# Three edits in the last stage of a fused attention and two-layer MLP kernel: a group of output stores ahead of weight loads, two VectorE steps exchanged, eight semaphores made four

## The chip, the cores and the metric

One core of a Trainium2 chip. The metric is the device time of one launch in microseconds (us), the median of some runs. In the profile PE is TensorE (PEld its weight loads), DVE is VectorE, ACT is ScalarE, POOL is GpSimd and SP is SyncE, which here only issues DMAs.

## The reference

All arrays are float32. Attention with a soft cap feeds a leaky MLP, which feeds a gated MLP with an RMS norm:

```python
# q, k, v: (2, 12, 448, 64)
scores = cap * np.tanh((q @ k.T) / np.sqrt(64) / cap)
attn = softmax(scores) ; x = (attn @ v) as (896, 768)
h = x @ w_in                                   # 768 -> 2048
x = np.maximum(0.01 * h, h) @ moe_w_out        # 2048 -> 768
xn = x / sqrt(mean(x * x, -1) + 1e-6) * rms_g
g, val = xn @ w_gate, xn @ w_val               # 768 -> 1536 each
out = (g * sigmoid(g) * val) @ w_out2          # 1536 -> 768
```

## The kernel before

Activations are kept transposed (features on the 128 partitions, the 448 tokens of one batch element in a row). Each product of a pair of weight row blocks with the two batch elements is done by a seven-product scheme of the Strassen kind: products named P1, P5, P7, P6, P3, P2 and P4, each on a half of the contraction. Every float32 product is made of three matmuls on a high and a low part of each operand (`w_hi` with `z_high`, `w_hi` with `z_low`, `w_lo` with `z_high`). One product of the last stage is so 3 x 3 = 9 matmuls of 128x128 weights on 448 columns.

The way of a weight: SP loads a raw block of 384 KB into one of four slots `w_raw` (`load_raw`); a slot is free when GpSimd has made the low part of the last weight that uses the old block (`raw_free`, a wait on `w_lo_done`). Products P1, P2 and P4 use the raw block as it is. The others use a sum or difference that DVE makes in `s_sum` (`s_part`, lines 1018 to 1027). ACT copies the weight to `w_hi` (line 686), GpSimd subtracts it from the original into `w_lo` (line 576), and PE waits for `w_lo_done` before the product. There are seven slots for finished weights.

The last stage, out = act @ w_out2, has three units, called `UNITS`, `UNITS + 1` and `UNITS + 2` in the code, and first, second and third unit here. Each makes two row blocks of the output for both batch elements. The second and the third have 14 products (seven for each half of the 1536 features); they use the banks of PSUM by turns, the third those of the first. DVE drains a unit by `take_p5`, `take_p7` and `take_p6` and by four results, `result_11`, `result_12`, `result_21` and `result_22`, in the buffers `sq0`, `sq1`, `u2` and `a_t`, from which SP stores them (`store`, line 551, 224 KB each).

Every engine runs its instructions in the order in which the code writes them, and the DMAs of loads and stores are all issued from SP, whose waits are in that same order: a DMA behind a wait is not issued before the wait is over. Nothing moves them at build time. `load_last(s)` issues a unit's four raw blocks (`w_raw` slots 0, 1, 2, 3), and before the change the end of SP's order is `load_last` of the three units and then `store` of the three. `z_lower(1, T4)` is three subtractions for the low part of the operand of the second unit's very last product (P4 of the second half). PE's order of a 14-product unit is P1, P5, P7, P6, the same four for the second half, and then P3, P2 and P4 (P3, P4 and P2 in the third unit), each for both halves.

Of the kernel before, what the change touches and what calls it, by code (L numbers as in the profile page):

```python
# [11 lines left out]
def at_least(eng, sem, value):  # L12

    if value > 0:
        eng.wait_ge(sem, value)


def build(nc, qk, v, cap, w_in, w_out, w_gate, w_val, w_out2, rms_g, out, recips):
    PAIRS, _, QK = qk.shape
# [8 lines left out]
    KH = KD // 2  # L28
# [13 lines left out]
    B11, T1, T3, T2, B22, B21, T4, B12 = range(8)  # L42
# [3 lines left out]
    UNITS = U1 + N2  # L46
# [29 lines left out]
    def raw_of(s):  # L76
        if s >= UNITS:
            return RAW_LAST + 4 * (s - UNITS)
        return 2 * s if s < U1 else 2 * U1 + STEPS // 2 + 2 * (s - U1)
# [10 lines left out]
    with ExitStack() as ctx:  # L90
# [71 lines left out]
        def sem(name):  # L162
            return ctx.enter_context(nc.semaphore(name))
# [10 lines left out]
        recip_out = sem("recip_out")  # L174
        recip_row_in = [sem(f"recip_row_in{s}") for s in range(2)]
        raw_in = [sem(f"raw_in{s}") for s in range(4)]
        out_sem = [[sem(f"out_stored{s}_{u}") for u in range(2)] for s in range(4)]

        ident_done = sem("ident_done")
        consts = sem("consts")  # L180
# [70 lines left out]
        def cols(i, n=S):  # L251
            return slice(i * n, i * n + n)

        def tiles(t, n):
            return t.rearrange("p (t c) -> p t c", c=n)
# [163 lines left out]
        O11, O12, O21, O22 = range(4)  # L419
# [41 lines left out]
        @block.sync  # L461
        def _(sp):
            def load_qk(p):

                at_least(sp, qk_hi_done, p - 1)
                at_least(sp, qk_lo_done, p - 1)
                c = slice(FIRST if p == 0 else 0, QK)
                sp.dma_start(qk_raw[p % 2][:, c], qk[p][:, c]).then_inc(qk_in[p % 2], 16)

            def load_v(p):  # L470

                at_least(sp, pv_done, p - 1)
                if p < 2:
                    sp.wait_ge(v_ones_set, p + 1)
                sp.dma_start(tiles(v_ones[p % 2][:, :], 128)[:, :, 0:D], v[p]).then_inc(v_in[p % 2], 16)

            def spread_sums(p):

                sp.wait_ge(x_raw_done, p + 1)
                at_least(sp, eps_done, p - 1)  # L480
                sp.dma_start(sums[p % 2][:, :],
                             x_raw[p % 2][D:D + 1, :].rearrange("o (p j) -> o p j", p=128)).then_inc(sums_in, 16)

            def store_recip(p):
                sp.wait_ge(recip_done, p + 1)
                sp.dma_start(recips[p].rearrange("(p j) -> p j", p=128), recip[p % 2][:, :]).then_inc(recip_out, 16)

            def load_recip_row(p):

                sp.wait_ge(recip_out, 16 * (p + 1))  # L490
                at_least(sp, x_norm_done, 2 * (p - 1))
                sp.dma_start(recip_row[p % 2][HEAD[0], :],
                             recips[p].partition_broadcast(D)).then_inc(recip_row_in[p % 2], 16)

            def raw_free(r):

                if RAW_OUT <= r < raw_of(U1):
                    sp.wait_ge(w_lo_done, W_OUT + 2 * (r - RAW_OUT) + 2)
                elif r < RAW_LAST:
                    s = r // 2 if r < RAW_OUT else U1 + (r - raw_of(U1)) // 2  # L500
                    sp.wait_ge(w_lo_done, widx(s, P4) + 1)
                else:
                    s, k = divmod(r - RAW_LAST, 4)
                    last = [(P2, 0), (P4, 0), (PB, 1), (PD, 1)][k] if s == 0 else ((P2, P4)[k % 2], k // 2)
                    sp.wait_ge(w_lo_done, widx(UNITS + s, *last) + 1)

            def load_raw(r, src):
                if r >= 4:
                    raw_free(r - 4)
                n = src.shape[-1]  # L510
                sp.dma_start(w_raw[r % 4][:, 0:n], src).then_inc(raw_in[r % 4], 16)

            sp.dma_start(qk_raw[0][:, 0:FIRST], qk[0][:, 0:FIRST]).then_inc(first_in, 16)
            load_qk(0)
            sp.wait_ge(first_in, 16)
            load_v(0)
            load_qk(1)
            load_qk(2)
            load_v(1)
            load_qk(3)  # L520
            for p in range(PAIRS):
                spread_sums(p)
                if p + 2 < PAIRS:
                    load_v(p + 2)
                if p + 4 < PAIRS:
                    load_qk(p + 4)
                if p < 4:
                    load_raw(p, w_in[p])
                store_recip(p)
                load_recip_row(p)  # L530
            sp.dma_start(rms_col[:, :], rms_g.rearrange("(c p) -> p c", p=128),
                         allow_slow_non_contiguous=True).then_inc(gains_in, 16)
            for r in range(4, RAW_OUT):
                load_raw(r, w_in[r])
            for k in range(STEPS // 2):
                load_raw(RAW_OUT + k, w_out[k])
            for f in range(N2):
                load_raw(raw_of(U1 + f), w_gate[f])
                load_raw(raw_of(U1 + f) + 1, w_val[f])

            def load_last(s):
                m, r = s - UNITS, raw_of(s)
                for k, (row, part) in enumerate(((m, 0), (m + KH, 0), (m, 1), (m + KH, 1))):
                    load_raw(r + k, w_out2[row, part])

            def store(s):
                for kind in RESULTS[s - UNITS]:
                    row, b, tile, scaled = result(s, kind)
                    row = s - UNITS + KH * row
                    sp.wait_ge(scaled, s - UNITS + 1)  # L550
                    sp.dma_start(out[row * 128:(row + 1) * 128, cols(b)], tile[:, :]).then_inc(out_sem[kind][(s - UNITS) % 2], 16)

            load_last(UNITS)
            load_last(UNITS + 1)
            load_last(UNITS + 2)
            store(UNITS)
            store(UNITS + 1)
            store(UNITS + 2)
            for kind in range(4):
                sp.wait_ge(out_sem[kind][0], 32)  # L560
                sp.wait_ge(out_sem[kind][1], 16)

        @block.gpsimd
        def _(pool):
# [375 lines left out]
        def _(dve):  # L940
# [95 lines left out]
            def take_p5(s):  # L1036

                dve.wait_ge(p1_kept, s + 1)
                dve.wait_ge(prod_done, count[widx(s, P5, last_part(s))])
                if s == LAST - 1:  # L1040
                    dve.wait_ge(out_sem[O22][0], 16)
                dve.tensor_tensor(a_t[s % 2][:, :], bank(s, BANK_C), p1[s % 2][:, :], ALU.add).then_inc(a_done, 1)

            def take_p7(s):

                dve.wait_ge(a_done, s + 1)
                dve.wait_ge(prod_done, count[widx(s, P7, last_part(s))])
                dve.tensor_tensor(a_t[s % 2][:, :], bank(s, BANK_D), a_t[s % 2][:, :], ALU.add).then_inc(a2_done, 1)

            def take_p6(s):  # L1050
                dve.wait_ge(prod_done, count[widx(s, P6, last_part(s))])
                if s == LAST - 1:
                    dve.wait_ge(out_sem[O21][0], 16)
                dve.tensor_tensor(u2[s % 2][:, :], bank(s, BANK_B), p1[s % 2][:, :], ALU.add).then_inc(u2_done, 1)


# [267 lines left out]
            def z_lower(part, blk):  # L1324
                for c in range(KH):
                    z_lo(part, blk, c)
# [12 lines left out]

            def result_11(s):  # L1340
                dve.wait_ge(act_done, 2 * N2)
                if s > UNITS:
                    dve.wait_ge(out_sem[O11][(s - 1 - UNITS) % 2], 16)
                wait_result(s, P2, PB)
                dve.tensor_tensor(sq[0][:, :], bank(s, BANK_A), r_bc[:, cols(0)], ALU.mult).then_inc(o11_done, 1)

            def result_12(s):
                dve.wait_ge(act_done, 2 * N2)
                dve.wait_ge(u2_done, s + 1)
                if s > UNITS:  # L1350
                    dve.wait_ge(out_sem[O12][(s - 1 - UNITS) % 2], 16)
                wait_result(s, P3, PB)
                dve.tensor_tensor(sq[1][:, :], bank(s, BANK_C), u2[s % 2][:, :], ALU.add).then_inc(c12_done, 1)
                dve.wait_ge(c12_done, s + 1)
                dve.tensor_tensor(sq[1][:, :], sq[1][:, :], r_bc[:, cols(1)], ALU.mult).then_inc(o12_done, 1)
# [15 lines left out]
            s = U1  # L1371
# [40 lines left out]
            s = UNITS - 1  # L1412
# [19 lines left out]
            s = UNITS  # L1432
# [22 lines left out]
            s_part(s + 1, P3, 1)  # L1455
            take_p5(s + 1)
            take_p7(s + 1)
            take_p6(s + 1)
            z_lower(1, T4)
            result_11(s)  # L1460
            result_12(s)
            result_21(s)
# [1 line left out]
            s = UNITS + 1  # L1464
# [8 lines left out]
            s = UNITS + 2  # L1473
# [362 lines left out]
```

## Time and profile before

| | us |
|---|---|
| three runs | 566.59, 568.21, 570.43 |
| median | 568.21 |
| profiled execution, its own time | 568.21 |
| its span in the profile | 566.4 |
| PE busy in the span | 561.6 |

The span is what the engines and queues show. The profiled execution took 568.21 us, 1.8 us more than its span, and it is also the median. So a time predicted from the trace is the span's change added to 568.21. The rows below use times from the start of the span. A group of an answer that merges several instructions (x3) shows one duration from the first one's start to the last one's end.

### The profile page before, as it was taken

How to read it: one execution, taken by the hardware profiler on the slowest of the kernel's cores; microseconds unless marked ns; L12 is line 12 of the kernel's file. 1: busy time of each engine (PE TensorE's matmuls, PEld its weight loads, DVE VectorE, ACT ScalarE, POOL GpSimd, SP SyncE). 2: the span in 40 equal slices, each digit the busy share in tenths (PEclk: the TensorE clock that was granted, in tenths of full speed). 3: DMA queues.
4: the chain of work that ended last, by engine and by line, in shares of the span. 5: the costliest groups of instructions: out<-in, count | busy, mean ns of one | idle time of the engine just before them, and what ended most of it. 6: DMA issues, size and time to landing. Idle time of an engine off the chain costs nothing.

```text
span 566.4 us, 7857 instructions
## 1 busy us (share of the span) xinstructions
PE 561.6 (99%) x2706; PEld 472.0 (83%) x2706; DVE 413.7 (73%) x575; ACT 294.4 (52%) x513; POOL 313.8 (55%) x272
## 2 busy tenths in 40 slices
PE   9999999999999999999999999999999999999997
PEld 5544554688999999999999999999999999998896
DVE  4468897685545455324985499999999999999963
ACT  6889888226444464434644456444334445825330
POOL 1026464479656652234853469767766897526672
PEclk9999999999999999999999999999999999999999
DMA  6355332123111142110211011111221111120511
GB/s 171 97 174 162 110 113 52 49 57 112 57 56 57 56 130 66 57 45 23 75 54 57 1 57 57 56 57 56 77 89 59 56 57 58 56 57 0 171 73 65
DMA packets 29720, 41.49 MB, mean 73 GB/s; under 512 B 17009, under 2 KB 18673, under 8 KB 29681
## 3 DMA queue, kind: packets, MB, share of 16 engines
q1 hardware_dynamic: 29536, 40.99, 23.0%
q8 instruction: 22, 0.36, 0.3%
q14 instruction: 18, 0.14, 0.1%
q10 hardware_dynamic: 144, 0.00, 0.0%
HBM read 38.15 MB, written 2.80 MB: 72 GB/s over the span
## 4 chain that ended last, share of the span: by engine, by line
PE 91%; DVE 4%; issue 3%; DMA 1%; ACT 0%; POOL 0%; DVEq 0%; ACTq 0%
PE ps L1579 46%; PE ps L1646 21%; PE ps L1514 9%; PE ps L1743 8%; PE ps L1502 4%; PE ps L1520 2%; PE ps L1506 1%; DVE act_lo L1321 1%; DVE x_lo L1321 1%; PE ps L1588 1%; DMA sums<-x_raw 1%; DVE x_raw L955 0%; DVE s_sum L1024 0%; POOL w_lo L576 0%; PE ps L1698 0%
## 5 line engine op out<-in xcount | busy, mean ns | idle before, releaser
L576 POOL TENSOR_TENSOR w_lo<-w_raw,w_hi 128x384 fp32r<-128x384 f32 x111 | 131.1, 1189 | 140.3 <-ACT w_hi L686 139.6
L1579 PE MATMUL ps<-x_hi,w_hi 128*128 128x448 f32 x420 | 154.9, 369 | 0.0
L1579 PE MATMUL ps<-x_hi,w_lo 128*128 128x448 f32 x420 | 154.1, 367 | 0.0
L1579 PE MATMUL ps<-x_lo,w_hi 128*128 128x448 f32 x420 | 154.0, 367 | 0.0
L576 POOL TENSOR_TENSOR w_lo<-s_sum,w_hi 128x384 fp32r<-128x384 f32 x100 | 113.6, 1149 | 69.5 <-ACT w_hi L686 69.5
L686 ACT ACTIVATE w_hi<-s_sum 128x384 fp32r<-128x384 f32 x100 | 51.2, 523 | 91.6 <-PE ps L1579 53.3
L1579 PEld LDWEIGHTS ps<-x_hi,w_hi 128*128 128x128 f32 x420 | 79.0, 188 | 8.4 <-issue 1.3
L1579 PEld LDWEIGHTS ps<-x_hi,w_lo 128*128 128x128 f32 x420 | 78.9, 188 | 7.0
L1579 PEld LDWEIGHTS ps<-x_lo,w_hi 128*128 128x128 f32 x420 | 79.0, 188 | 6.7
L686 ACT ACTIVATE w_hi<-w_raw 128x384 fp32r<-128x384 f32 x111 | 56.3, 514 | 11.8 <-PE ps L1579 7.2
L1514 PE MATMUL ps<-probs,v_ones 128*65 128x448 f32 x144 | 56.6, 541 | 0.2 <-DVE x_raw L955 0.2
L662 ACT ACTIVATE probs<-ps,capc 128x896 f32<-128x896 f32 (+1 forms) x48 | 42.0, 901 | 12.2 <-PE ps L1502 10.8
L1514 PEld LDWEIGHTS ps<-probs,v_ones 128*65 128x65 f32 x144 | 19.3, 137 | 30.3 <-issue 29.1
L669 ACT ACTIVATE probs<-probs,capc 128x1344 f32<-128x1344 f32 (+2 forms) x25 | 41.1, 1644 | 0.8
L1132 DVE TENSOR_TENSOR x_lo<-g,x_hi 128x448 fp32r<-128x448 f32 x32 | 22.1, 736 | 23.5 <-ACT x_hi L718 23.5
L1132 DVE TENSOR_TENSOR ring_lo<-g,ring_hi 128x448 fp32r<-128x448 f32 x32 | 24.6, 812 | 15.2 <-ACT ring_hi L718 15.2
L1027 DVE TENSOR_TENSOR s_sum<-w_raw,s_sum 128x384 f32<-128x384 f32 x25 | 26.2, 1049 | 5.7 <-POOL w_lo L576 3.5
L1743 PE MATMUL ps<-act_lo,w_hi 128*128 128x448 f32 x84 | 29.9, 368 | 0.0
L1018 DVE TENSOR_TENSOR s_sum<-w_raw 128x384 f32<-128x384 f32 x25 | 23.2, 929 | 7.4 <-DMA w_raw<-in_w_in 6.4
L718 ACT ACTIVATE ring_hi<-g 128x448 fp32r<-128x448 f32 x32 | 16.6, 569 | 22.5 <-PE ps L1646 22.5
L718 ACT ACTIVATE x_hi<-g 128x448 fp32r<-128x448 f32 x32 | 16.6, 570 | 21.8 <-PE ps L1646 21.8
L1646 PE MATMUL ps<-ring_hi,w_lo 128*128 128x448 f32 x96 | 27.5, 368 | 0.0
(182 smaller groups left out, 1047.2 us busy)
## 6 DMA issues: line engine op xcount, KB each, us to landing
w_raw<-in_w_out SPq DMA_DIRECT2D x28, 384.0 KB, 3.1
w_raw<-in_w_in SPq DMA_DIRECT2D x16, 384.0 KB, 3.8
qk_raw<-in_qk SPq DMA_DIRECT2D x11, 480.0 KB, 4.3
w_raw<-in_w_gate SPq DMA_DIRECT2D x12, 384.0 KB, 3.0
w_raw<-in_w_val SPq DMA_DIRECT2D x12, 384.0 KB, 3.6
v_ones<-in_v SPq DMA_DIRECT2D x12, 224.0 KB, 3.3
recip_row<-recips SPq DMA_DIRECT2D x12, 224.0 KB, 3.3
out<-sq SPq DMA_DIRECT2D x6, 224.0 KB, 1.9
```

The costliest lines, as they stand in the source:

```text
L576: pool.tensor_tensor(w_lo[:, c], source, w_hi[:, c].bitcast(F32), ALU.subtract).then_inc(w_lo_done, 1)
L662: act.activation(tiles(probs_of(p, i, n), S), ps[:, bank_of(p, i):bank_of(p, i) + n, 0:S], ACT.Tanh, scale=capc[:, 4:5]).then_inc(tanh_don ...
L669: act.activation(c, c, ACT.Exp, scale=capc[:, 2:3], bias=capc[:, 6:7]).then_inc(exp_done, 1)
L686: act.activation(w_hi[:, c], w_source(n), ACT.Copy).then_inc(w_hi_done, 1)
L718: act.activation(ring(i, b, ring_hi, x_hi), g_tile(2 * f + b), ACT.Copy).then_inc(g_hi_done, 1)
L1018: dve.tensor_tensor(dst, m2[:, lower], m2[:, upper], ALU.add).then_inc(s_done, 1)
L1027: dve.tensor_tensor(dst, m1[:, upper], s_sum[:, cols(2, HALF)], ALU.subtract).then_inc(s_done, 1)
L1132: dve.tensor_tensor(ring(i, b, ring_lo, x_lo), g_tile(2 * f + b), ring(i, b, ring_hi, x_hi).bitcast(F32), ALU.subtract).then_inc(g_lo_done, 1)
L1514: pe.matmul(ps[0:D + 1, pv_bank(p) + h, 0:S], v_ones[p % 2][:, c:c + D + 1], probs[p % 2][:, (2 * t + h) * S:(2 * t + h + 1) * S], start=( ...
L1579: last = pe.matmul(ps[:, base(s) + BANK_OF[j], 0:S], w[:, w_c], x[:, xs(j, c)], start=(j in (P1, P5, P7, P6) and c == 0 and w is w_hi and ...
L1646: last = pe.matmul(ps[:, ROW_BANK[m] + b, 0:S], w[:, w_c], ring(i, b, beside, in_x), start=(f == 0 and w is w_hi and x == "hi"), stop=(f = ...
L1743: last = pe.matmul(ps[:, base(s) + BANK_OF[j], 0:S], w[:, w_c], x(part, j, c), start=(j in (P1, P5, P7, P6) and part == 0 and c == 0 and w ...
```

## The change

1. In SP's order, `store(UNITS)`, the four output stores of the first unit, now stands between `load_last(UNITS + 1)` and `load_last(UNITS + 2)`, ahead of the third unit's four raw loads.
2. In DVE's order, `z_lower(1, T4)` now stands before `take_p6(s + 1)`.
3. The semaphores of the stores, two for each of four kinds of result, are one for each kind, which counts up; the waits are for 16, 32 or 48 on it, and the last one of SP is four waits, where it was eight.

```diff
-        out_sem = [[sem(f"out_stored{s}_{u}") for u in range(2)] for s in range(4)]
+        out_sem = [sem(f"out_stored{s}") for s in range(4)]
...
-                    sp.dma_start(out[row * 128:(row + 1) * 128, cols(b)], tile[:, :]).then_inc(out_sem[kind][(s - UNITS) % 2], 16)
+                    sp.dma_start(out[row * 128:(row + 1) * 128, cols(b)], tile[:, :]).then_inc(out_sem[kind], 16)
...
             load_last(UNITS)
             load_last(UNITS + 1)
+            store(UNITS)
             load_last(UNITS + 2)
-            store(UNITS)
             store(UNITS + 1)
             store(UNITS + 2)
             for kind in range(4):
-                sp.wait_ge(out_sem[kind][0], 32)
-                sp.wait_ge(out_sem[kind][1], 16)
+                sp.wait_ge(out_sem[kind], 16 * KH)
...
                 if s == LAST - 1:
-                    dve.wait_ge(out_sem[O22][0], 16)
+                    dve.wait_ge(out_sem[O22], 16 * (s - 1 - UNITS))
...
                 if s == LAST - 1:
-                    dve.wait_ge(out_sem[O21][0], 16)
+                    dve.wait_ge(out_sem[O21], 16 * (s - 1 - UNITS))
...
             def result_11(s):
                 dve.wait_ge(act_done, 2 * N2)
-                if s > UNITS:
-                    dve.wait_ge(out_sem[O11][(s - 1 - UNITS) % 2], 16)
+                at_least(dve, out_sem[O11], 16 * (s - UNITS))
...
             take_p7(s + 1)
+            z_lower(1, T4)
             take_p6(s + 1)
-            z_lower(1, T4)
             result_11(s)
```

SP's queue near its end, the change against the kernel before. `w_raw_51` to `w_raw_54` are the raw slots 0 to 3 (the first two rows end the second unit's loads, the unmarked four are the third unit's), `sq_67`, `sq_68`, `u_0_62` and `a_t_60` hold the first unit's results 11, 12, 21 and 22:

```order
 L511 DMA w_raw_53<-in_w_out 128x768
 L511 DMA w_raw_54<-in_w_out 128x768
+L551 DMA out<-sq_67 128x448
+L551 DMA out<-sq_68 128x448
+L551 DMA out<-u_0_62 128x448
+L551 DMA out<-a_t_60 128x448
 L511 DMA w_raw_51<-in_w_out 128x768
 L511 DMA w_raw_52<-in_w_out 128x768
 L511 DMA w_raw_53<-in_w_out 128x768
 L511 DMA w_raw_54<-in_w_out 128x768
-L551 DMA out<-sq_67 128x448
-L551 DMA out<-sq_68 128x448
-L551 DMA out<-u_0_62 128x448
-L551 DMA out<-a_t_60 128x448
```

The four stores moved ahead of the four loads; each store has a wait for its own result.

DVE's order in the second unit, before, from `take_p5` of the second unit (line 1042) over the results of the first to the first weight sum of the third unit (line 1018):

```order
L1042 TENSOR_TENSOR a_t_61<-ps,p_1_59 128x448 [waits prod_done,p1_kept]
L1048 TENSOR_TENSOR a_t_61<-ps,a_t_61 128x448 [waits prod_done,a_done]
L1054 TENSOR_TENSOR u_1_63<-ps,p_1_59 128x448 [waits prod_done]
L1321 TENSOR_TENSOR act_lo<-act_full,x_lo 128x448 [waits z_hi_done] x3
L1345 TENSOR_TENSOR sq_67<-ps,r_bc 128x448 [waits prod_done,act_done]
L1353 TENSOR_TENSOR sq_68<-ps,u_0_62 128x448 [waits prod_done,u2_done,act_done]
L1355 TENSOR_TENSOR sq_68<-sq_68,r_bc 128x448 [waits c12_done]
L1359 TENSOR_TENSOR u_0_62<-ps,u_0_62 128x448 [waits prod_done]
L1361 TENSOR_TENSOR u_0_62<-u_0_62,r_bc 128x448 [waits c21_done]
L1366 TENSOR_TENSOR a_t_60<-ps,a_t_60 128x448 [waits prod_done,a2_done]
L1368 TENSOR_TENSOR a_t_60<-a_t_60,r_bc 128x448 [waits c22_done]
L1018 TENSOR_TENSOR s_sum<-w_raw_52 128x384 [waits raw_in1,w_lo_done]
```

The same place in the changed kernel (its line numbers are one to three lower):

```order
L1041 TENSOR_TENSOR a_t_61<-ps,p_1_59 128x448 [waits prod_done,p1_kept]
L1047 TENSOR_TENSOR a_t_61<-ps,a_t_61 128x448 [waits prod_done,a_done]
L1320 TENSOR_TENSOR act_lo<-act_full,x_lo 128x448 [waits z_hi_done] x3
L1053 TENSOR_TENSOR u_1_63<-ps,p_1_59 128x448 [waits prod_done]
L1343 TENSOR_TENSOR sq_67<-ps,r_bc 128x448 [waits prod_done,act_done]
```

The three subtractions stand one place earlier, `take_p6` three places later; from `result_11` on, nothing moved.

## Rows read from the trace of the kernel before

**Rows 1.** The page's head and busy times by engine, whole span

```profile
span 566.4 us, 7857 instructions
...
PE 561.6 (99%) x2706; PEld 472.0 (83%) x2706; DVE 413.7 (73%) x575; ACT 294.4 (52%) x513; POOL 313.8 (55%) x272
```

**Rows 2.** Chain that ended last, from 524 us: start, duration, what

```profile
524.09 39.22 PE ps L1743 x189
...
563.43 0.62 DVE sq L1345
```

**Rows 3.** Timeline, PE: first matmul of second and third unit, last matmul

```profile
510.60 0.37 PE L1743 MATMUL ps<-z_ring,w_hi 128*128 128x448 f32 x1
...
537.28 0.37 PE L1743 MATMUL ps<-z_ring,w_hi 128*128 128x448 f32 x1
...
562.92 0.37 PE L1743 MATMUL ps<-x_hi,w_lo 128*128 128x448 f32 x1
```

**Rows 4.** Timeline, SP's DMA issues from 525 to 536 us

```profile
528.64 4.01 SPq L511 DMA_DIRECT2D w_raw<-in_w_out  x4
532.70 0.91 SPq L551 DMA_DIRECT2D out<-sq  x2
534.16 0.33 SPq L551 DMA_DIRECT2D out<-u  x1
535.35 0.33 SPq L551 DMA_DIRECT2D out<-a_t  x1
```

**Rows 5.** Line 511 alone: first load (528 to 529 us), other three (530 to 567)

```profile
L511 SPq DMA_DIRECT2D w_raw<-in_w_out x1: 328/328/328, 528.6 to 528.6; - x1
...
DMA to landing us min/median/max: 3.0/3.0/3.0
...
L511 SPq DMA_DIRECT2D w_raw<-in_w_out x3: 327/328/433, 531.4 to 532.3; - x3
...
DMA to landing us min/median/max: 3.0/3.6/4.6
```

**Rows 6.** Timeline, ACT and POOL: weights from 526 to 541 us

```profile
531.75 0.53 ACT L686 ACTIVATE w_hi<-w_raw 128x384 fp32r<-128x384 f32 x1 [3.99 <-DMA w_raw<-in_w_out]
535.89 1.46 ACT L686 ACTIVATE w_hi<-s_sum 128x384 fp32r<-128x384 f32 x3 [3.61 <-DVE s_sum L1018]
...
527.16 6.49 POOL L576 TENSOR_TENSOR w_lo<-w_raw,w_hi 128x384 fp32r<-128x384 f32 x5
536.49 3.76 POOL L576 TENSOR_TENSOR w_lo<-s_sum,w_hi 128x384 fp32r<-128x384 f32 x3 [2.84 <-ACT w_hi L686]
540.22 1.39 POOL L576 TENSOR_TENSOR w_lo<-w_raw,w_hi 128x384 fp32r<-128x384 f32 x1
```

**Rows 7.** Line 576 alone, 531.9 to 536.4 and 536.4 to 540.2 us: min/median/max ns

```profile
L576 POOL TENSOR_TENSOR w_lo<-w_raw,w_hi x2: 1018/1158/1298, 531.3 to 532.4; 128x384 fp32r<-128x384 f32 x2
...
L576 POOL TENSOR_TENSOR w_lo<-s_sum,w_hi x3: 1113/1322/1397, 536.5 to 538.9; 128x384 fp32r<-128x384 f32 x3
```

**Rows 8.** Timeline, DVE from 526 to 549 us

```profile
526.59 0.62 DVE L1054 TENSOR_TENSOR u<-ps,p 128x448 f32<-128x448 f32 x1
527.12 3.33 DVE L1321 TENSOR_TENSOR act_lo<-act_full,x_lo 128x448 fp32r<-128x448 f32 x3
...
531.54 1.23 DVE L1355 TENSOR_TENSOR sq<-sq,r_bc 128x448 f32<-128x448 f32 x1
532.70 0.61 DVE L1359 TENSOR_TENSOR u<-ps,u 128x448 f32<-128x448 f32 x1
533.35 0.79 DVE L1361 TENSOR_TENSOR u<-u,r_bc 128x448 f32<-128x448 f32 x1
534.05 0.61 DVE L1366 TENSOR_TENSOR a_t<-ps,a_t 128x448 f32<-128x448 f32 x1
534.70 0.62 DVE L1368 TENSOR_TENSOR a_t<-a_t,r_bc 128x448 f32<-128x448 f32 x1
535.24 0.55 DVE L1018 TENSOR_TENSOR s_sum<-w_raw 128x384 f32<-128x384 f32 x1
...
548.79 0.56 DVE L1027 TENSOR_TENSOR s_sum<-w_raw,s_sum 128x384 f32<-128x384 f32 x1 [3.48 <-POOL w_lo L576]
```

**Rows 9.** Stretches: busy us by engine (count), granted clock, DMA share, GB/s

```profile
526.00:537.30 11.30, 11.30 (x56) 10.28 (x56) 11.06 (x17) 3.70 (x10) 8.23 (x7) 1.00 0.58 186
537.30:563.30 26.00, 25.99 (x127) 23.49 (x125) 14.30 (x21) 5.07 (x12) 14.08 (x13) 1.00 0.21 79
```

**Rows 10.** Waits of PE, whole span: total us, times, longest us

```profile
PE ps L1588 <- DVE extra L1083: 1.1, 1, 1.1
PE ps L1743 <- DVE act_lo L1321: 0.4, 1, 0.4
```

More of the change, by code:

```diff
@@ L1349, in result_12 @@
                 dve.wait_ge(u2_done, s + 1)
-                if s > UNITS:
-                    dve.wait_ge(out_sem[O12][(s - 1 - UNITS) % 2], 16)
+                at_least(dve, out_sem[O12], 16 * (s - UNITS))
                 wait_result(s, P3, PB)
```

## The prediction

> **What bounds the kernel now.** I read the page's busy times first: PE is busy for 561.6 of 566.4 us [rows 1], so whatever leaves PE's stream unbroken costs nothing, and whatever breaks it is paid in full. The chain that ended last says the same of the place of the change: from 524.09 us it is one unbroken run of PE, then one DVE result and its store [rows 2]. PE's waits are 1.1 us at the start and 0.4 us near 524 us [rows 10]. So the question is whether any edit makes PE wait, or takes one of these small waits away. For that I read the timeline of each engine around the border of the second and the third unit. The third unit starts at 537.28 us [rows 3]; from there to its last matmul at 562.92 it has 126 matmuls, one each (562.92 - 537.28) / 125 = 0.205 us, and a product of nine takes 1.85 us. In this stretch PE has 25.99 of 26 us busy [rows 9].
>
> **Part 1, the stores ahead of the loads.** Follow the third unit's first weight. Before, SP issued its raw load at 528.64 [rows 4], it took 3.0 us to land [rows 5], so 531.64; ACT, which had stood 3.99 us waiting for just this, copied it from 531.75 to 532.28, and GpSimd ended the low part, the last of a group of five, at 527.16 + 6.49 = 533.65 [rows 6]. PE needed it at 537.28. The cover is 537.28 - 533.65 = **3.63 us**, and it is all that the load may lose.
>
> Now the load stands behind four stores, each with a wait for its result. The last of them, result 22, is ended by DVE at 534.70 + 0.62 = 535.32 [rows 8] and its store is issued at 535.35 for 0.33 us [rows 4]. The first load can then be issued at 535.68, which is 535.68 - 528.64 = **7.04 us** later. That the stores' own issue is early matters little: before, the first two stood ready while SP was still at its loads, which ended at 528.64 + 4.01 = 532.65, but nobody needed them then. Of the loads all four are late, and the first is only the first one to be missed.
>
> What DVE does does not depend on these loads until the weight sum at 535.24, behind result 22 [rows 8], so the time of result 22 stays nearly what it is. PE's stall follows: 7.04 - 3.63 = 3.41 us. Three corrections. (a) Against it: GpSimd took 1.30 us for this weight (the longer of the two in the first row of [rows 7], as the ACT copy's end at 532.28 and the group's end place it), with DVE busy beside it; then DVE will be waiting too, and the quick case is 1.02 us [rows 7], so -0.28. (b) Against it: without this GpSimd step at 532.4 to 533.65, DVE's steps beside it may be shorter; line 1361 took 0.79 us there and line 1355 took 1.23, where the undisturbed line 1368 of the same shape takes 0.62 [rows 8]. The first is worth 0.17 and little of the second stays free of GpSimd's earlier step; I take -0.1, bound -0.4. (c) For it: the load starts right behind two stores. The three loads that were issued within 1 us of each other landed after 3.0, 3.6 and 4.6 us [rows 5], so sharing the DMA engines costs up to 1.6 us; a store is 224 KB to a load's 384, and the one directly ahead is 0.33 us ahead, so I take +0.4, bound 0 to 1.6. Sum: 3.41 - 0.28 - 0.1 + 0.4 = 3.43, so **3.4 us**, between 2.7 (both gains whole and no contention) and 5.0.
>
> Is a later weight worse? The second product, P5, needs the second load and DVE's sum. Before, DVE's sum at 535.24 led to a finished weight at about 536.49 + 1.3 = 537.8 (GpSimd) [rows 6, 7], 2.55 us on. Now the second load is issued at about 536.0, lands 3.6 us on (the middle value of rows 5) at 539.6, and the weight is ready at 539.7 + 2.5 = 542.2. PE, starting P1 at 537.28 + 3.4 = 540.7, asks for it at 540.7 + 1.85 = 542.55. So it is just covered, by 0.3 us; if it isn't, the rest adds to the stall and is inside the 5.0 above. P7 and P6 follow at GpSimd's pace of 3.76 / 3 = 1.25 us each [rows 6] against PE's 1.85, so they gain on PE. The sums of the second half come behind results of the second unit in DVE's queue; these are late by about as much as DVE waited (539.7 - 535.24 = 4.5 us), PE by 3.4, and DVE has an idle 3.48 us before 548.79 [rows 8] to catch up. So there is one stall, at the start of the third unit, and everything behind it, the last result and the last store, moves by it.
>
> What does the move give? The first unit's stores land earlier by up to some us, and `take_p5`, `take_p6` and the results of the later units wait for them to have landed. DVE's row at 548.79 names a GpSimd weight as its releaser, and no row of DVE in this stretch names a store [rows 8]; the gain is nothing.
>
> **Part 2, the exchange on DVE.** `take_p6` ran at 526.59 with no idle ahead, then the three subtractions from 527.12 to 530.45 [rows 8]. DVE is busy for 11.06 of the 11.3 us to 537.30 [rows 9], so there is no idle time for the exchange to fill: three subtractions 0.5 us earlier, `take_p6` some 3.3 us later, and `result_11` at the same time. The subtractions are needed by the second unit's last product, at 537.28 - 1.85 = 535.4, 5 us after their end either way. The later `take_p6` is read only by results of the second unit and keeps a bank that nobody writes again. 0 us; were DVE to wait there, it would be at most the 0.6 us of one step, and it would be hidden too.
>
> **Part 3, the semaphores.** The same stores are waited for at the same places. Four waits fewer at SP's end, when all but the last store are long down: no row prices one, but DVE finished at 563.43 + 0.62 = 564.05 [rows 2] and the span closed at 566.4 [rows 1], so all of the store, its landing and the eight waits is 2.35 us, and half of the waits can't be more than a few tenths of it. I take 0, bound -0.4.
>
> **Sum.** 568.21 + 3.4 = **571.6 us**, from the profiled execution, which is also the median of the three runs. It is +0.6%: a measurement of this kernel can hardly tell less than 1% from no change, so this counts as within 1% (up to 573.9 us).
>
> **The rivals.**
> *No stall, so not slower* (568.1 us, chance 0.07). The mechanism would be DVE: if result 22 were ended early enough, SP would be at the loads in time. The point from which it decides is 3.63 + 0.28 us of cover: result 22 would have to be done by 535.32 - 7.04 + 3.91 = 532.2, 3.1 us sooner. Against it: DVE is full from 526 to 537.3 [rows 9] and works off the same instructions; the largest gain that rows show is the 0.4 us of (b). For it speaks only that a part of the cover might be hidden in how the trace places an end.
> *A lower clock after the stall* (573.4 to 575.3, I say 574.4; chance 0.10). In this trace the granted clock of every stretch is 1.00, the 2.4 GHz level, but PE's longest wait in it is 1.1 us [rows 9, 10], so it has no row after a stall like this one. The stall predicted is three times as long. If TensorE came back at 1.2 GHz, a product would take 3.7 instead of 1.85 us, and each product done so adds 1.85; one or two of them make 1.85 to 3.7 us on top of the 3.4. I give it little, since the 1.1 us wait shows no trace of it.
> The Trainium skill (TensorE: Matmul & The Clock Gate, section Part 1: The HAM clock gate) says that an idle TensorE falls to half its rate and must work for some us before it gets the full rate back; by that rule this change would cost its stall and a slow start of the third unit as well. No row of this trace bears it out or speaks against it.
> *A deeper stall from the DMAs* (573.5, chance 0.12). The loads share the engines with two stores and with each other, and both P1 and then P5 come late: 4.6 us landing for the first, and P5 beyond its 0.3 us cover. That is 5.0 us plus up to 0.5. For it: the DMA share in 526 to 537.3 is already 0.58 [rows 9]. Against it: the first of the three bunched loads still landed in 3.0 us.
> *Something else in the run* (chance 0.03), of either sign, such as a part 2 that releases something that I don't see.
>
> **How the numbers follow.** The forecast, one stall of 2.7 to 5.0 us at the third unit's start, has 0.68. Its bounds give 570.9 to 573.2. The three runs before spread from 566.59 to 570.43, -1.6 and +2.2 us about the median, and a comparison of medians keeps perhaps half of that. The range is 569.6 to 575.0: on the low side the forecast's lower bound less 1.3, on the high side the clock rival's upper end nearly whole. It leaves out the no-stall case and little else. Slower by over 1% needs more than 5.7 us: most of the clock rival and a part of the deeper stall, 0.13. Faster by over 1%: 0.02. Within 1%: 0.85.
>
> **What would show it.** In the changed kernel's timeline SP should have four stores, the last at about 535.2, then four loads from about 535.6 to 537; ACT an idle stretch before the third unit's first weight that ends near 539 and names the raw load; PE a wait of 3.4 us near 537.3 that names GpSimd's `w_lo`, and no second one over 0.5 us; DVE an idle stretch of 4 us or so before line 1017, where it had none; the last matmul near 566.3 and a span near 569.8. The granted clock behind the stall tells the second rival. The prediction is wrong if PE's wait is under 2.5 us or over 5, or if the exchange on DVE shows a wait of PE in the second unit.

## The result and the profile after

| | before | changed |
|---|---|---|
| median of 8 runs, us | 567.5 | 572.54 |
| lowest to highest | 566.19 to 570.43 | 571.49 to 575.61 |
| profiled execution, its time | 568.21 | 572.8 |
| its span | 566.4 | 571.0 |

The ratio is 1.0095, with a 95% interval of 1.0066 to 1.0124: slower by 5.0 us between the medians, 5.4 us by the ratio. The forecast was 571.6 (569.6 to 575.0).

The waits of PE in the changed kernel, longest first (total us, times, longest us), to be held against [rows 10]:

```profile
PE ps L1740 <- POOL w_lo L575: 3.1, 1, 3.1
PE ps L1585 <- DVE extra L1082: 1.1, 1, 1.1
PE ps L1499 <- DVE qk_lo L1079: 0.5, 1, 0.5
PE ps L1740 <- DVE act_lo L1320: 0.4, 1, 0.4
```

One long wait is new: 3.1 us for a weight's low part. (The 0.5 us for `qk_lo` belongs to an early stage that the change doesn't touch; it is 0.2 us in the profile of the exchange alone.) The timeline of SP, ACT and POOL around it, the counterpart of [rows 4, 6]:

```profile
530.12 1.61 SPq L551 DMA_DIRECT2D out<-sq  x2
532.57 0.33 SPq L551 DMA_DIRECT2D out<-u  x1
533.77 0.33 SPq L551 DMA_DIRECT2D out<-a_t  x1
534.14 1.88 SPq L511 DMA_DIRECT2D w_raw<-in_w_out  x4
...
537.50 0.52 ACT L685 ACTIVATE w_hi<-w_raw 128x384 fp32r<-128x384 f32 x1 [11.12 <-DMA w_raw<-in_w_out]
...
538.10 0.99 POOL L575 TENSOR_TENSOR w_lo<-w_raw,w_hi 128x384 fp32r<-128x384 f32 x1 [7.23 <-ACT w_hi L685]
```

Four stores, the last of them at 533.77 when result 22 is done, and right behind it the four loads. Before, the first of the loads was issued 537.28 - 528.64 = 8.64 us before PE wanted its product [rows 3, 4]. PE, in its own timeline,

```profile
535.67 0.37 PE L1740 MATMUL ps<-x_lo,w_lo 128*128 128x448 f32 x1
539.14 0.74 PE L1740 MATMUL ps<-z_ring,w_hi 128*128 128x448 f32 x1 [3.11 <-POOL w_lo L575]
539.68 0.57 PE L1740 MATMUL ps<-act_lo,w_hi 128*128 128x448 f32 x1
540.06 0.57 PE L1740 MATMUL ps<-z_ring,w_lo 128*128 128x448 f32 x1
...
544.54 0.57 PE L1740 MATMUL ps<-z_ring,w_lo 128*128 128x448 f32 x1
544.91 0.41 PE L1740 MATMUL ps<-z_ring,w_hi 128*128 128x448 f32 x1
545.16 0.36 PE L1740 MATMUL ps<-act_lo,w_hi 128*128 128x448 f32 x1
545.36 0.37 PE L1740 MATMUL ps<-z_ring,w_lo 128*128 128x448 f32 x1
```

wanted it one matmul after 535.67, at 535.88, and the load was issued at 534.14, 1.74 us before that. So the load lost 8.64 - 1.74 = 6.90 us of its lead. Its way from issue to the finished low part took 538.10 + 0.99 - 534.14 = 4.95 us, about as before (533.65 - 528.64 = 5.01 [rows 4, 6]); PE started 0.05 us later.

The second thing in these rows is the spacing of the matmuls behind the wait: 0.37 us instead of 0.205, from 539.14 to 544.91, and then 0.20 again. The stretches of the wait, the slow matmuls and the rest (busy us of PE, PEld, DVE, ACT and POOL with counts, granted clock, DMA share, GB/s) answer to [rows 9]:

```profile
535.90:539.14 3.24, 0.14 (x1) 0.00 (x0) 0.65 (x1) 0.52 (x1) 0.99 (x1) 0.85 0.98 378
539.14:544.91 5.77, 5.76 (x15) 5.12 (x16) 5.60 (x9) 1.87 (x4) 4.71 (x4) 0.50 0.22 86
544.91:567.90 22.99, 22.97 (x112) 20.70 (x110) 10.44 (x16) 4.60 (x10) 10.15 (x10) 1.00 0.17 61
```

The granted clock is 0.50, the 1.2 GHz level, in the second row; it fell while PE was idle (the 0.85 of the first row is a mean) and came back at 544.91, with PE at work. PE looks fully busy in this stretch (5.76 of 5.77 us), so its busy share does not tell of the loss; the count does, 15 matmuls in 5.77 us.

The sum for this execution uses one measure, also below: the gap at the unit's start beyond the 0.205 us of one matmul, and the distance from the unit's first matmul to its last, which was 25.64 us before [rows 3]. The gap is 539.14 - 535.67 - 0.205 = 3.27 us. The distance is 567.51 - 539.14 = 28.37 us, 2.73 us longer. Together 6.0 us. The span grew by only 4.6, since in this execution the third unit was due 1.4 us earlier (535.88, not 537.28). That start moved from 535.5 to 538.2 us among the profiled executions of this study, with the change and without it. That is as much as the spread between runs of one kernel and may be a part of it; no kernel was profiled twice, so this isn't shown.

### The profile page after: what moved, and what is told of

Its sections match the earlier page's. It is cut to its first block, busy times and chain, and to the rows that moved or that the text cites. A ratio compares the mean times of both kernels' runs of the same rounds, so it can differ in the third digit from the quotient of the medians.

```text
span 571.0 us, 7855 instructions
## 1 busy us (share of the span) xinstructions
PE 562.5 (99%) x2706; PEld 473.5 (83%) x2706; DVE 415.2 (73%) x575; ACT 294.3 (52%) x513; POOL 313.6 (55%) x272
## 4 chain that ended last, share of the span: by engine, by line
PE 92%; DVE 4%; DMA 2%; issue 1%; POOL 0%; ACT 0%; SPq 0%; DVEq 0%; ACTq 0%
PE ps L1576 45%; PE ps L1643 21%; PE ps L1740 10%; PE ps L1511 8%; PE ps L1499 3%; PE ps L1757 3%; PE ps L1517 2%; PE ps L1503 1%; DVE act_lo L1320 1%; DVE x_raw L954 1%; DMA qk_raw<-in_qk 1%; DMA w_raw<-in_w_out 1%; DMA sums<-x_raw 1%; DVE s_sum L1023 0%; DVE sums_eps L960 0%
```

## The experiments

Each ran beside the kernel before on the same chip: the first four below share one (kernel before 568.03 us), the last four another (567.52 us). Code lines with + and - stand against the kernel that is named.

**Only the stores moved.** Against the kernel before:

```diff
             load_last(UNITS + 1)
+            store(UNITS)
             load_last(UNITS + 2)
-            store(UNITS)
```

> The kernel before with the first unit's four stores ahead of the third unit's loads, and nothing else. Theory A (late loads make PE wait, and the wait costs the clock as well): the wait of about 3.1 us for GpSimd's low part at the third unit's start, then some 15 matmuls at 0.373 us instead of 0.205 (+2.5 us), together +5 to +6 us over before, as the full change (+5.0 between medians). Theory B (the exchange on VectorE or the merged semaphores carry a part of it): clearly less than the full change, by 1 us or more.

Measured: 572.14 us against 568.03, ratio 1.0078 (1.0055 to 1.0101), so +4.4 us (3.1 to 5.7). In the profile a gap of 539.50 - 535.79 - 0.205 = 3.51 us and a distance of 27.13 us (+1.49): 5.0 us. The granted clock fell late in the wait and was back at 542.93:

```profile
536.00:539.50 3.50, 0.16 (x1) 0.00 (x1) 0.72 (x1) 0.52 (x1) 0.99 (x1) 0.98 0.96 375
539.50:542.93 3.43, 3.43 (x10) 3.09 (x10) 3.29 (x6) 1.87 (x4) 2.38 (x3) 0.52 0.12 49
542.93:567.00 24.07, 24.07 (x118) 21.79 (x116) 12.81 (x19) 4.61 (x10) 12.51 (x12) 1.00 0.18 68
```

The slow stretch is 9 matmuls here, not 15. The move alone carries the change, within the interval: +4.4 us to the full change's +5.4, whose intervals overlap. The mean clocks of the six executions were 0.994, 0.997 (three), 0.999 and 1.0, so in one or two of them the clock seems not to have fallen; these two took 571.76 and 572.37 us, no less than the rest.

**Only the exchange on DVE.** Against the kernel before:

```diff
             take_p7(s + 1)
+            z_lower(1, T4)
             take_p6(s + 1)
-            z_lower(1, T4)
```

> The kernel before with the three subtractions ahead of take_p6, and nothing else. Theory A: no difference from before within 0.3%, no wait of PE over 0.5 us in the second unit, clock 1.00. Theory B: slower by 1 us or more, or an idle stretch of VectorE that was not there.

Measured: 567.64 against 568.03 us, ratio 0.9993 (0.9974 to 1.0012), no new wait of PE in the last stage, mean clock 1.0 in the profile. The exchange is worth nothing that this resolves. The merged semaphores were not tried by themselves; the run with two loads first, below, has them.

**The wait filled.** Against the changed kernel, ahead of the third unit's products:

```diff
             for s in range(UNITS + 1, LAST):
+                if s == UNITS + 2:
+                    pe.wait_ge(o11_done, 1)
+                    for _ in range(4):
+                        pe.matmul(ps[:, base(s) + BANK_A, 0:S], ident[:, :], r_bc[:, cols(0)], start=True, stop=True)
```

> The changed kernel; while PE would wait for the third unit's first weight, it runs four float32 matmuls of the identity with the inverse-norm tile into the bank that the unit is going to clear (about 0.75 us each, 3 us), whose result is thrown away. Theory A (stall and clock are two separate costs, 3.1 us and 2.7 us): the stall remains, filled, the clock stays at 1.00 and the matmuls behind it at 0.205 us; +3.0 to +3.8 us over before, 1.7 to 2.7 us under the changed kernel. Theory B (the slow matmuls behind the stall come from something else at that place, such as the loads' DMA traffic or the busy SBUF): they stay slow, and the time is that of the changed kernel or worse.

The waits are still there, but PE has work in them (stretch of the filling, stretch of the unit):

```profile
538.15:541.49 3.34, 3.17 (x9) 1.33 (x7) 0.69 (x1) 0.52 (x1) 0.99 (x1) 1.00 0.96 338
541.49:567.90 26.41, 26.29 (x126) 23.50 (x126) 16.05 (x24) 6.48 (x14) 14.88 (x13) 1.00 0.20 74
```

No slow matmul, clock 1.00, with loads, DVE and POOL behind the wait as busy as before: it is the idle PE that takes the clock down, and not the traffic at that place. The mean clock of all six executions was 0.999 or 1.0. Measured: 572.28 us, ratio 1.0068 (1.0045 to 1.0091), +3.9 us. The profile's sum is 541.49 - 537.94 - 0.205 = 3.35 us of gap and a distance of 567.63 - 541.49 = 26.14 us (+0.50), 3.85. But the saving against the stores moved alone (572.14 us, same chip) doesn't show in the medians; the expected 1.7 to 2.7 us under the changed kernel came out as 1.5 by the ratios (1.0095 to 1.0068), in separate measurements and with intervals that overlap. So this run shows the mechanism and leaves the price open; the pair below gives it.

It also shows something that the slow clock had hidden:

```profile
543.24 0.36 PE L1740 MATMUL ps<-z_ring,w_lo 128*128 128x448 f32 x1
543.72 0.47 PE L1740 MATMUL ps<-z_ring,w_hi 128*128 128x448 f32 x1
544.03 0.37 PE L1740 MATMUL ps<-act_lo,w_hi 128*128 128x448 f32 x1
```

The second product, P5, starts 0.27 us late (0.48 instead of 0.205) and its second matmul 0.1 late. P1's second matmul was 0.1 late too; together this is the 0.50. With P1 at half rate, P5's weight comes in time.

**Two loads first, then the stores.** Against the changed kernel, where `load_last` takes the blocks that it issues:

```diff
+            load_last(UNITS + 2, range(2))
             store(UNITS)
-            load_last(UNITS + 2)
+            load_last(UNITS + 2, range(2, 4))
```

> The changed kernel with two of the third unit's four loads ahead of the first unit's stores and two behind (exchange and merged semaphores stay). Theory A: the first four products need only the first two loads, the third load, 3 us earlier issued than PE needs it through ACT and GpSimd, comes in time; no wait of PE at the third unit, time that of before within 0.3%. Theory B (stores and loads share the DMA engines, and their order does not matter so much as that they stand together): a wait remains, +1 us or more.

Measured: 567.32 against 568.03 us, ratio 0.9989 (0.9975 to 1.0003). The gap at the unit's start is gone and the distance is 561.43 - 535.79 = 25.64 us, that of the kernel before. So four stores ahead of the last two loads cost nothing; it is which load stands behind them. This run also has the exchange and the merged semaphores, so all three together are worth between -1.4 and +0.2 us once no load is late. The slack is visible in ACT, which waits 1.84 us for the third load and is still early for PE, whose fifth product is due at 535.79 + 4 x 1.85 = 543.2:

```profile
534.20 0.93 SPq L511 DMA_DIRECT2D w_raw<-in_w_out  x2
...
537.66 0.53 ACT L687 ACTIVATE w_hi<-w_raw 128x384 fp32r<-128x384 f32 x1 [1.84 <-DMA w_raw<-in_w_out]
```

**One load first.** As the last, with `range(1)` and `range(1, 4)`.

> The changed kernel with one of the third unit's loads ahead of the first unit's stores and three behind. Theory A (a product waits by what its own load is late beyond its cover): no wait for the first product; the second, P5, waits: its load is issued about 4.3 us later than in the kernel before, against a cover of 1.4 us between GpSimd's end and PE's start, some of it given back by quicker steps, so 2 to 3 us of wait, at the second product. Theory B (PE's wait comes from the loads standing in one burst): still 3 us at the first product. The clock: the wait is 2 to 3 us; if it falls, the total is +3 to +5 us, if it stays, +2 to +3 us.

Measured: 570.69 against 567.52 us, ratio 1.0071 (1.0043 to 1.0098), +4.0 us. The first product ran on time and the wait came at the second:

```profile
539.57 0.37 PE L1742 MATMUL ps<-z_ring,w_lo 128*128 128x448 f32 x1
542.37 0.47 PE L1742 MATMUL ps<-z_ring,w_hi 128*128 128x448 f32 x1 [2.43 <-POOL w_lo L577]
542.68 0.49 PE L1742 MATMUL ps<-act_lo,w_hi 128*128 128x448 f32 x1
542.97 0.57 PE L1742 MATMUL ps<-z_ring,w_lo 128*128 128x448 f32 x1
```

That is 2.6 us of gap in the unit, and its distance is 29.88 us, 4.24 more, so 1.6 us are the clock's. Here it fell only when PE was at work again, between the second and the third matmul, as the stretches show (wait, first three matmuls, the next ten):

```profile
539.57:542.37 2.80, 0.37 (x3) 0.00 (x1) 2.30 (x4) 1.75 (x4) 1.15 (x2) 1.00 0.53 195
542.37:543.00 0.63, 0.63 (x3) 0.57 (x4) 0.63 (x2) 0.12 (x1) 0.63 (x1) 0.81 0.00 0
543.00:546.00 3.00, 3.00 (x10) 2.65 (x9) 2.93 (x5) 0.00 (x0) 3.00 (x3) 0.50 0.21 76
```

**The loads behind the last store's landing.** Against the changed kernel:

```diff
             store(UNITS)
+            sp.wait_ge(out_sem[O22], 16)
             load_last(UNITS + 2)
```

> The changed kernel, and SP waits until the store of result 22 has landed (about 2 us) before it issues the third unit's loads. Theory A: PE's wait grows by 1.5 to 2 us to about 5 us; the clock falls in it as in the changed kernel and is low for some us behind it (at least nine matmuls at 0.373 us), so +6.5 to +8 us over before. Theory B (the length of the slow stretch grows with the wait): over 15 slow matmuls and +8.5 us or more.

Measured: 574.06 against 567.52 us, ratio 1.0124 (1.0101 to 1.0147), +7.0 us. The gap is 542.27 - 537.21 - 0.205 = 4.86 us, the distance 569.90 - 542.27 = 27.63 us (+1.99), sum 6.85. The wait is 1.6 us longer than in the changed kernel and the slow stretch shorter (11 matmuls), so in these profiles its length doesn't grow with the wait:

```profile
542.27:546.50 4.23, 4.23 (x11) 3.84 (x12) 4.09 (x7) 1.87 (x4) 3.17 (x3) 0.50 0.13 53
```

The stores had all landed when these loads were issued (each within 2.0 us, the last issued at 535.29, the loads from 537.26), and still the first load took 3.3 us:

```profile
DMA to landing us min/median/max: 3.3/4.2/4.9
```

**The same, filled.** Six matmuls in place of four, in that kernel.

> As the run with the loads behind the landing of the store, with six float32 matmuls of the identity in the wait of PE (about 4.6 us), whose result is thrown away. Theory A: no slow matmul of the products behind, P5's own wait shows for up to 0.5 us, and the time is 1 to 2.5 us under that of the same kernel without them. Theory B (the clock costs nothing net): the same time as that.

Measured: 572.57 us, ratio 1.0092 (1.007 to 1.0114), +5.2 us, 1.5 us under the same kernel without the filling (medians, same chip). The profile gives 541.71 - 536.74 - 0.205 = 4.77 us of gap and 567.78 - 541.71 = 26.07 us of distance (+0.43), 5.2. All six executions without the filling had a mean granted clock of 0.994 or 0.997, all six with it 0.999 or 1.0. The stretch of the unit's products in its profile:

```profile
541.70:568.00 26.30, 26.17 (x126) 23.51 (x126) 16.13 (x24) 6.47 (x14) 14.91 (x13) 1.00 0.19 71
```

The intervals of the two ratios still touch, but the two kernels can be held against each other directly, six executions each: the means are 574.24 and 572.52 us, 1.7 us apart (95% interval 0.6 to 2.9), and the profiles' sums differ by 6.85 - 5.2 = 1.65 us. So the lower clock cost some 1.5 to 1.7 us there.

**Two stores ahead.** Against the kernel before, where `store` takes the kinds that it issues:

```diff
             load_last(UNITS + 1)
+            store(UNITS, slice(0, 2))
             load_last(UNITS + 2)
-            store(UNITS)
+            store(UNITS, slice(2, 4))
```

> The kernel before with only two of the first unit's stores (results 11 and 12) ahead of the third unit's loads, two behind. Theory A: the first load is issued when result 12 is done, about 3.9 us later than before (stores at about 531 and 532, load at 532.6 on the clock of the trace before), against a cover of 3.6 us: PE waits for 0 to 0.8 us, the clock stays, and the time is that of before within 0.3%. Theory B (any move of stores ahead of the loads costs by their share of the DMA engines): half of the full change or more, +2.5 us.

Measured: 568.8 against 567.52 us, ratio 1.0026 (1.0008 to 1.0044), +1.5 us. The wait was 1.42 us where 0 to 0.8 was expected. The loads were issued 4.1 us before PE's demand, so 4.55 us late, not 3.9, and the first took 3.9 us to land, not 3.0:

```profile
529.20 2.14 SPq L551 DMA_DIRECT2D out<-sq  x2
531.38 1.88 SPq L511 DMA_DIRECT2D w_raw<-in_w_out  x4
```

The landing of the four loads, from the view of line 511 alone:

```profile
DMA to landing us min/median/max: 3.9/5.0/6.1
```

The clock stayed (0.999 in the profile; 0.999 or 1.0 in all ten executions), and no matmul was slow. The gap is 1.58 us and the distance 26.04 (+0.40, mostly P5's lateness again), 2.0 together.

All of it in one table (us). "Sum" is the profile's gap and added distance, "measured" the ratio times the median of before.

| order at SP | first late product | gap | distance over 25.64 | sum | measured |
|---|---|---|---|---|---|
| two loads first | none | 0 | 0 | 0 | -0.6 |
| two stores ahead | P1 | 1.58 | 0.40 | 2.0 | +1.5 |
| one load first | P5 | 2.6, within the unit | 4.24 in all | 4.2 | +4.0 |
| stores ahead, wait filled | P1 | 3.35 | 0.50 | 3.9 | +3.9 |
| stores ahead | P1 | 3.51 | 1.49 | 5.0 | +4.4 |
| the changed kernel | P1 | 3.27 | 2.73 | 6.0 | +5.4 |
| after the landing, filled | P1 | 4.77 | 0.43 | 5.2 | +5.2 |
| after the landing | P1 | 4.86 | 1.99 | 6.9 | +7.0 |

## Why the prediction was right, and where not

The direction, the place and the way were right, and the time lay in the range; the likeliest case was not what happened. What happened is the rival that had 0.10, the lower clock after the stall. That the median, 572.54, lies even between the bounds of the forecast without it (570.9 to 573.2) is luck: these bounds were made wide for a DMA contention that cost almost nothing, and the clock's cost fell into that room.

*What bounds the kernel, and one stall at the third unit's start.* Right: PE has one new wait, at the first product, which names GpSimd's low part.

*The stall's size, 7.04 - 3.63 = 3.41, corrected to 3.4.* Right: the load lost 6.90 us of its lead and the gap is 3.27. The corrections had the right sign and cancel: GpSimd took 0.99 us and not 1.30 (-0.31, priced -0.28); the first load was issued 1.74 us before PE's demand, where 537.28 - 535.68 = 1.60 was forecast (-0.14, priced -0.1); and the first load's landing took 0.25 us more (priced +0.4; issue 534.14, ACT at 537.50, where it was 528.64 and 531.75 [rows 4, 6]). The reason given for the last, the stores ahead, isn't what the runs show: with all stores landed the first of the four loads also took 3.3 us. The load read as 3.0 was issued 2.8 us ahead of the next one; these four came within 1.5 us.

*P5 covered by 0.3 us.* Wrong by 0.6 or so: in all three profiles with a late P1 and the full clock, P5 started 0.27 us late. Two terms were too small. In the run with the changed kernel's wait filled, the sum began 541.49 - 540.80 = 0.69 us before P1's start, where 1.0 was forecast; and from there to the finished weight it took 2.87 us, where 2.55 was read: the sum alone took 1.05 us, overlapping GpSimd's step for P1, and not 0.55 [rows 8]. In the changed kernel the slow first product covers it, so the step's error doesn't reach the time. The DVE wait of 4.75 us before the sum was forecast as 4.5.

*The exchange and the semaphores at nothing.* The exchange: right, shown by the run of it alone. The semaphores: not run by themselves, but the kernel with two loads first has both edits and takes 0.9989 of the time before (0.9975 to 1.0003). So no run gives them a part of the 1.0 us between +4.4 and +5.4, which isn't resolved.

*The step that failed*, though the time lay in the range, is the clock's chance: "I give it little, since the 1.1 us wait shows no trace of it", and before it that the trace "has no row after a stall like this one". It was mis-sized, as a chance and not as a price: 2.73 us in the profiled execution, inside the 1.85 to 3.7 that the rival worked out, and 1.5 to 1.7 us in the pair with and without filling. All profiled and timed executions of the changed kernel had a mean clock of 0.994 or 0.997. By (1 - 0.997) x 571 / 0.5 the second is some 3.4 us at the lower level and the first 6.9; seven of the eight timed ones had 0.997. At 0.373 us for each matmul instead of 0.205, 3.4 us at the lower level cost at most 3.4 x (1 - 0.205 / 0.373) = 1.5 us (an estimate), so the profiled 2.73 is more than a usual execution's, and the median, 572.54, lies under the 573.4 at which the rival's range began. Why the wait of 1.1 us said nothing: it stands at the very start, where the clock was low already. The rows were in the trace of before, and I had not read them by their durations. PE's first matmuls and weight loads there (line 1588; min/median/max ns, first and last start):

```profile
L1588 PEld LDWEIGHTS ps<-extra x18: 286/333/334, 1.1 to 4.7; 128*128 128x128 f32 x18
```

A load of 128x128 weights took 333 ns there and 188 ns later in the kernel (PEld in its page's lines). One line shows the change by itself, with operands and shape unchanged:

```profile
6.14 0.57 PE L1502 MATMUL ps<-qk_hi,qk_lo 64*128 64x448 f32 x2
7.33 0.36 PE L1502 MATMUL ps<-qk_hi,qk_lo 64*128 64x448 f32 x2
```

The granted clock of the first stretch was given as 1.00 all the same (columns as in [rows 9]):

```profile
1.10:6.00 4.90, 4.90 (x22) 4.58 (x24) 1.60 (x6) 2.01 (x3) 1.69 (x4) 1.00 0.40 105
```

In the slow stretch of the changed kernel it takes 330 ns:

```profile
L1740 PEld LDWEIGHTS ps<-z_ring,w_hi x6: 287/330/330, 539.1 to 544.5; 128*128 128x128 f32 x6
```

So the trace did have a start at the lower rate, up to about 7 us, in durations and not in the clock column. That took away the only reason given for the rival's 0.10, and it deserved far more. How short a wait brings the lower rate, these rows don't say. The Trainium skill (TensorE: Matmul & The Clock Gate, Part 1: The HAM clock gate) says that an idle TensorE drops to half rate and is given the full rate again only after sustained work. The trace of the changed kernel agrees (granted clock 0.50 behind the wait, 1.00 after 5.77 us of matmuls).

*The gains from earlier stores, at nothing.* Right: with two loads ahead of the stores nothing waits and nothing is gained (0.9989, interval to 1.0003).

## What to carry to other kernels

In a queue that runs in order, ask of each DMA how much lead it has and not whether the queue is busy: here four stores that no product waits for took 6.9 us of a load's 8.6 us lead, and moving them behind the first two loads, whose products come first, made the cost vanish. Where PE bounds the kernel, a wait of PE can cost more than its length: here each of the four profiled waits of 2.4 us or more that PE spent idle also cost 1.5 to 2.7 us of half rate, and the wait of 1.4 us did not. And a first wait can hide a second one: price the next product by its own chain, at the full rate.

## What the runs showed of the hardware

- The granted clock went to its 1.2 GHz level in each profiled execution with an idle wait of PE of 2.4, 3.1, 3.3 and 4.7 us, and in none with 1.4 us or with the wait filled by matmuls. The fall can come late in the wait or, for the 2.4 us one, after PE has started again.
- The low level lasted for 9 to 15 matmuls of 448 columns behind the wait (3.3 to 5.8 us at 0.373 us each instead of 0.205), longest with the 3.1 us wait and not with the 4.7 us one. The fall is not in every execution: of the six with only the stores moved, two had a mean clock of 0.999 and 1.0. They took 571.76 and 572.37 us, no less than the others, which is not explained. And one of the 23 executions of the kernel before beside it had 0.997 (571.74 us), without the change.
- The granted clock read 1.00 in the first 6 us, though weight loads took 333 ns there, as long as at 0.50 later on in the changed kernel (330 ns). At the start of a trace the durations tell the rate, the clock column did not.
- A raw load of 384 KB took 3.0 us to land when the next one was issued 2.8 us later [rows 5]. As the first of a burst of four it took 3.3 us right behind the stores (changed kernel) and 3.3 us with all stores landed; the slowest of the four took 5.3 and 4.9 us. With two stores ahead of the burst and two right behind it, it was 3.9 and 6.1 us.
